# Numerators copied out of PSUM by ScalarE and divided by GpSimd, in an attention, mixture and FFN kernel on one core

## The reference

```
def phi(x):                                  # x: [4 batches, 8 heads, 576 tokens, 64]
    proj = einsum('bhsd,df->bhsf', x, w_phi) # 128 features
    proj = proj - max(abs(proj), -1)
    return concatenate([exp(proj), exp(-proj)], -1)
q_p, k_p = phi(q), phi(k)
kv, z = einsum('bhsf,bhsd->bhfd', k_p, v), sum(k_p, 2)
num = einsum('bhsf,bhfd->bhsd', q_p, kv)
den = einsum('bhsf,bhf->bhs', q_p, z) + 1e-6
x = num / den                                # 2304 tokens x 512
e = argmax(x @ w_gate)                       # one of 8 experts for each token
x = softmax weight * sigmoid(x @ w_output_gate)[e] * (relu(x @ w1[e]) @ w2[e])
x = x / rms(x) * rms_g
out = (silu(x @ w_gate2) * (x @ w_val)) @ w_out
```

## Time and profile before

| | us |
|---|---|
| runs | 900.57, 896.76, 899.69 (median 899.69) |
| the profiled execution | 903.42, span 901.8 |
| TensorE busy, matmuls | 874.1 (97% of the span) |
| VectorE busy | 432.3 (48%) |
| ScalarE busy | 294.0 (33%) |
| GpSimd busy | 123.2 (14%) |

### The profile page before, as it was taken

The page is one execution under the profiler, slowest core; times in us unless marked ns, Lnnn a source line. Parts: engine busy times, 40 slices in busy tenths (PEclk is TensorE's granted clock), DMA queues, the critical chain, the costliest instruction groups (busy, mean ns, idle before and its releaser), DMA issues.

```text
span 901.8 us, 16710 instructions
## 1 busy us (share of the span) xinstructions
PE 874.1 (97%) x6432; PEld 792.1 (88%) x6433; DVE 432.3 (48%) x875; ACT 294.0 (33%) x479; POOL 123.2 (14%) x145
## 2 busy tenths in 40 slices
PE   8999999998999999999999999999999999999996
PEld 6776858678999999999989999999999999999996
DVE  5687787988586444433457422222222222222222
ACT  4555444662255433223354221121121112112111
POOL 1010202023244211224300010010001001001001
PEclk9999999999999999999999999999999999999999
DMA  8614614012637443237633520030020002000000
GB/s 285 194 54 183 216 52 156 3 54 55 250 129 155 80 64 73 57 42 182 146 121 137 160 104 1 1 105 1 1 70 35 0 14 91 0 0 36 1 1 36
DMA packets 37185, 75.37 MB, mean 84 GB/s; under 512 B 8176, under 2 KB 24688, under 8 KB 35472
## 3 DMA queue, kind: packets, MB, share of 16 engines
q1 hardware_dynamic: 32832, 56.07, 23.0%
q0 software_dynamic: 3488, 17.85, 5.3%
q10 hardware_dynamic: 816, 0.79, 0.3%
HBM read 51.06 MB, written 23.64 MB: 83 GB/s over the span
## 4 chain that ended last, share of the span: by engine, by line
PE 83%; DVE 7%; DMA 4%; issue 3%; ACT 2%; POOL 0%; POOLq 0%; SPq 0%; DVEq 0%; ACTq 0%
PE ps L1026 10%; PE ps L1028 10%; PE ps L1027 10%; PE ps L1041 5%; PE ps L1042 5%; PE ps L1040 5%; PE ps L928 3%; PE ps L941 3%; PE ps L929 3%; PE ps L930 3%; PE ps L943 3%; PE ps L942 3%; PE ps L769 3%; PE ps L824 3%; PE ps L729 2%
## 5 line engine op out<-in xcount | busy, mean ns | idle before, releaser
L1026 PE MATMUL ps<-xnH,blkH 128*128 128x384 f32 x576 | 193.7, 336 | 3.0 <-DVE blkL L1693 1.9
L1028 PE MATMUL ps<-xnH,blkL 128*128 128x384 f32 x576 | 193.4, 336 | 0.0
L1027 PE MATMUL ps<-xnL,blkH 128*128 128x384 f32 x576 | 193.2, 335 | 0.0
L1700 DVE TENSOR_TENSOR sg<-sg,ps 128x384 f32<-128x384 f32 x72 | 39.8, 553 | 245.1 <-ACT sg L1259 245.1
L1259 ACT ACTIVATE sg<-ps 128x384 f32<-128x384 f32 x72 | 35.4, 491 | 251.8 <-PE ps L1028 251.8
L1026 PEld LDWEIGHTS ps<-xnH,blkH 128*128 128x128 f32 x576 | 108.2, 188 | 7.1 <-issue 4.4
L1027 PEld LDWEIGHTS ps<-xnL,blkH 128*128 128x128 f32 x576 | 108.2, 188 | 2.7
L1028 PEld LDWEIGHTS ps<-xnH,blkL 128*128 128x128 f32 x576 | 108.1, 188 | 0.0
L1041 PE MATMUL ps<-blkL,hH 128*128 128x512 f32 x216 | 84.8, 393 | 0.0
L1042 PE MATMUL ps<-blkH,hL 128*128 128x512 f32 x216 | 84.8, 392 | 0.0
L1040 PE MATMUL ps<-blkH,hH 128*128 128x512 f32 x216 | 84.5, 391 | 0.0
(11 more groups left out here) (219 smaller groups left out, 1553.8 us busy)
## 6 DMA issues: line engine op xcount, KB each, us to landing
stage<-in_ffn_w SPq DMA_DIRECT2D x12, 768.0 KB, 4.3
xin<-xs_dram SPq DMA_DIRECT2D x9, 578.2 KB, 9.5
xs_dram<-zrow SPq DMA_DIRECT2D x8, 578.2 KB, 8.6
qT<-in_q SPq DMA_DIRECT2D x4, 1152.0 KB, 5.8
xnH_dram<-xoH SPq DMA_DIRECT2D x8, 576.0 KB, 3.5
xnL_dram<-xoL SPq DMA_DIRECT2D x8, 576.0 KB, 5.4
xnH<-xnH_dram SPq DMA_DIRECT2D x6, 768.0 KB, 4.9
xnL<-xnL_dram SPq DMA_DIRECT2D x6, 768.0 KB, 6.3
```

Source lines behind the costliest of these rows:

```text
L1026: e.matmul(o, hi, xnH[par][:, c, :], start=(c == 0), stop=False)
L1027: e.matmul(o, hi, xnL[par][:, c, :], start=False, stop=False)
L1028: last = e.matmul(o, lo, xnH[par][:, c, :], start=False, stop=(c == KC - 1))
```

## The change

`x5` goes; `x5n` holds the 81 values of each head for two tiles, in SBUF, and `rd` becomes double, too. The four full tiles of a batch are copied out of PSUM by ScalarE; the packed tile by VectorE. GpSimd multiplies by the reciprocal where it copied before. Each tile waits until the tile two before it has been divided. The early step's flag comes one slot earlier, its rows are loaded once the last batch's key projections (not its query projections) are through, and GpSimd gates them between Q0 and Q1 of the last batch.

```diff
+            def copy_numerators(at):                      # ScalarE
+                j = at[1] % NJ
+                e.wait_ge(s["pe_N"], nkq(at))
+                if not (isinstance(at[0], int) and at[0] == 0 and j < 2):
+                    e.wait_ge(s["pool_x"], aside_of(two_before(at)))
+                    e.wait_ge(s["dve_lp"], nkq(two_before(at)))
+                e.activation(x5n[:, j % 2, :, :].rearrange("p (b h) e -> p b (h e)", b=2),
+                             num_of(at).rearrange("p b h e -> p b (h e)"), ACT.Copy)\
+                    .then_inc(s["act_N"], 1)
...
             def slot(b, sl):                              # ScalarE
...
+                g2 = before_slot(b, sl, 2)
+                full = is_q(g2) and not packed(g2)
+                if full and is_q(g1):
+                    copy_numerators(g2)
                 if is_k(g1):
...
                 if is_q(g1):
...
                     e.wait_ge(s["pe_pT"], nkq(g1))
                     e.activation(ex[:, g1[1] % 2, 0, heads, :], PMT[:, heads, :], ACT.Exp)
                     e.activation(ex[:, g1[1] % 2, 1, heads, :], PMT[:, heads, :], ACT.Exp, scale=-1.0)\
                         .then_inc(s["act_Q"], 1)
+                if full and not is_q(g1):
+                    copy_numerators(g2)
...
             def normalise(at):                            # VectorE
+                if not (isinstance(at[0], int) and at[0] == 0 and j < 2):
+                    e.wait_ge(s["pool_x"], aside_of(two_before(at)))
+                if packed(at):
+                    e.wait_ge(s["pe_N"], nkq(at))
+                    e.wait_ge(s["dve_lp"], nkq(two_before(at)))
+                    e.tensor_copy(x5n[:, j % 2, 0:HALF, :], num_of(at)[:, 0, :, :]).then_inc(s["dve_N"], 1)
+                    e.wait_ge(s["dve_N"], at[0] + 1)
+                else:
+                    e.wait_ge(s["act_N"], nfull(at))
...
-                e.tensor_tensor(x5[:, j, 0:heads * D].rearrange("p (b h d) -> p b h d", b=banks, d=D),
-                                num[:, :, :, 0:D], r4.unsqueeze(3).to_broadcast([P, banks, 4, D]), ALU.mult)\
-                    .then_inc(s["dve_N"], 1)
...
             def set_aside(b, j):                          # GpSimd
-                e.wait_ge(s["dve_N"], b * NJ + (j + 1))
+                e.wait_ge(s["dve_rd"], nkq(at) * 2)
-                    e.tensor_copy(x5s[0:n, j, 0:DM], x5[0:n, j, :]).then_inc(s["pool_x"], 1)
+                    e.tensor_tensor(x5s[:, j, 0:DM].rearrange("p (h d) -> p h d", d=D), x5n[:, j % 2, :, 0:D],
+                                    rd[:, j % 2, :].unsqueeze(2).to_broadcast([P, H, D]), ALU.mult)\
+                        .then_inc(s["pool_x"], 1)
...
-            for j in range(2):
-                set_aside(B - 1, j)
+            set_aside(B - 1, 0)
             e.wait_ge(s["r_early"], 1)
             with e.If(early > 0):
                 gate_rows(0)
-            for j in range(2, NJ):
+            for j in range(1, NJ):
                 set_aside(B - 1, j)
...
-                e.wait_ge(s["pe_P"], B * 2 * NS)          # SyncE, ahead of the early rows
+                e.wait_ge(s["pe_P"], (B - 1) * (2 * NS) + 2 * NJ)
...
-                    e.wait_ge(s["dve_N"], at[0] * NJ - 1) # TensorE, ahead of a batch's first key sums
+                    e.wait_ge(s["act_N"], at[0] * (NJ - 1))
-                        e.wait_ge(s["dve_N"], nkq((at[0], at[1] - 2)))  # and of numerators
+                        e.wait_ge(s["act_N"], nfull((at[0], at[1] - 2)))
...
-                if isinstance(b, int) and (b, sl) == (B - 1, 8):        # VectorE
+                if isinstance(b, int) and (b, sl) == (B - 1, 7):
                     route_early()
```

More of the change, by code:

```diff
@@ L96, in build_program @@
         kvs = att("kvs", [P, KC, 4, VA])
-        x5 = att("x5", [P, NJ, DM])
+        x5n = att("x5n", [P, 2, H, VA])
         x5s = att("x5s", [P, NJ, ROW])
@@ L171, in build_program @@
         mx = sb("mx", [P, 2, H])
-        rd = sb("rd", [P, H])
+        rd = sb("rd", [P, 2, H])
         lg = sb("lg", [P, NJ, 2 * E])
@@ L231, in build_program @@
                 "act_kv dve_kv pe_C act_cv dve_cv",
-            "queries: transposed, features, numerators, 1 / denominators, rows; logits by head, logits":
-                "pe_pT act_Q pe_N dve_rd dve_N dve_lp dve_g dve_L",
+            "queries: transposed, features, numerators, on chip, 1 / denominators; logits by head, logits":
+                "pe_pT act_Q pe_N act_N dve_N dve_rd dve_lp dve_g dve_L",
             "routing: steps, experts, exponentials, ranks, ranks read, places": "r_chain r_hot r_exp pe_R r_evac r_pos",
-            "rows set aside, scattered, their buffers free": "pool_x scat c_vec",
+            "rows normalised, scattered, their buffers free": "pool_x scat c_vec",
             "the early step's flag, its steps; the table": "r_early e_chain tab_set",
@@ L309, in nkq, with nfull @@
             return at[0] * NJ + (at[1] % NJ + 1)
+        def nfull(at):
+            return at[0] * (NJ - 1) + (at[1] % NJ + 1)
         def num_of(at):
@@ L314, in num_of, with two_before, aside_of @@
             return ps[:, first:first + 2, 0:4 * VA].rearrange("p b (h e) -> p b h e", e=VA)
+        def two_before(at):
+            j = at[1] % NJ
+            return (at[0], at[1] - 2) if j > 1 else (at[0] - 1, NS - 1 - j)
+        def aside_of(at):
+            return at[0] * (NJ + 1) + (NJ + 1 + at[1] % NJ + 1 + packed(at))
         def settle(eng, name):
@@ L591, in set_aside @@
             def set_aside(b, j):
-                n = rows_of(j)
-                e.wait_ge(s["dve_N"], b * NJ + (j + 1))
+                at = (b, NJ + j)
+                e.wait_ge(s["dve_rd"], nkq(at) * 2)
                 settle(e, "carry_pool")
-                if j < NJ - 1:
-                    e.tensor_copy(x5s[0:n, j, 0:DM], x5[0:n, j, :]).then_inc(s["pool_x"], 1)
-                else:
-                    e.wait_ge(s["pool_x"], b * (NJ + 1) + (NJ + 1 + j))
-                    settle(e, "carry_pool")
[L600 to L604, removed]
+                if not packed(at):
+                    e.tensor_tensor(x5s[:, j, 0:DM].rearrange("p (h d) -> p h d", d=D), x5n[:, j % 2, :, 0:D],
+                                    rd[:, j % 2, :].unsqueeze(2).to_broadcast([P, H, D]), ALU.mult)\
+                        .then_inc(s["pool_x"], 1)
+                    return
+                e.wait_ge(s["pool_x"], b * (NJ + 1) + (NJ + 1 + j))
+                settle(e, "carry_pool")
+                for g in range(2):
+                    rows = rows_half(g)
+                    e.tensor_tensor(x5s[0:REM, j, g * HALF * D:(g + 1) * HALF * D].rearrange("p (h d) -> p h d", d=D),
+                                    x5n[rows, j % 2, 0:HALF, 0:D], rd[rows, j % 2, 0:HALF].unsqueeze(2)
+                                    .to_broadcast([REM, HALF, D]), ALU.mult).then_inc(s["pool_x"], 1)
+                    e.wait_ge(s["pool_x"], b * (NJ + 1) + (NJ + 1 + j + 1 + g))
+                    settle(e, "carry_pool")
             def scatter(b):
@@ L772, in key_sums @@
                 if j == 0 and not first:
-                    e.wait_ge(s["dve_N"], at[0] * NJ)
+                    e.wait_ge(s["dve_N"], at[0])
                     settle(e, "carry_pe")
@@ L980, in _ @@
                 hidden(0, 0, 1)
-                e.wait_ge(s["dve_N"], B * NJ)
+                e.wait_ge(s["dve_N"], B)
                 hidden(0, 0, 2)
@@ L1095, in tile_high @@
                 e.activation(tH[sl % 2][:, :, 0:rows_of(sl % NJ)], tile_of(at), ACT.Copy).then_inc(s["act_x"], 1)
+            def copy_numerators(at):
+                j = at[1] % NJ
+                e.wait_ge(s["pe_N"], nkq(at))
[5 more added lines that the diff above has]
+                    .then_inc(s["act_N"], 1)
             def turned_evac(b, i):
@@ L1347, in normalise @@
             def normalise(at):
[L1348 to L1351, removed]
+                j, heads = at[1] % NJ, HALF if packed(at) else H
+                num, r = x5n[:, j % 2, 0:heads, :], rd[:, j % 2, 0:heads]
+                if not (isinstance(at[0], int) and at[0] == 0 and j < 2):
+                    e.wait_ge(s["pool_x"], aside_of(two_before(at)))
@@ L1352, in normalise @@
+                if packed(at):
[5 more added lines that the diff above has]
+                    e.wait_ge(s["act_N"], nfull(at))
                 if j > 0:
-                    e.wait_ge(s["dve_N"], nkq(at) - 1)
                     e.wait_ge(s["dve_L"], nkq(at) - 1)
@@ L1355, in normalise @@
                 links = (nkq(at) - 1) * 2
-                r4 = rd[:, 0:heads].rearrange("p (b h) -> p b h", b=banks)
-                e.tensor_scalar(r4, num[:, :, :, VW], 1e-6, None, ALU.add).then_inc(s["dve_rd"], 1)
+                e.tensor_scalar(r, num[:, :, VW], 1e-6, None, ALU.add).then_inc(s["dve_rd"], 1)
                 e.wait_ge(s["dve_rd"], links + 1)
-                e.reciprocal(rd[:, 0:heads], rd[:, 0:heads]).then_inc(s["dve_rd"], 1)
```

(6 more changed lines are left out.)

## The result

The changed kernel takes 932.66 us (median of 4 runs, 930.42 to 935.62), the kernel before 898.95: ratio 1.0378, 95% interval 1.0354 to 1.0402, slower by 33.7 us. The forecast was 923.8, in a range from 916 to 932: the sign was right, the loss over a quarter too small.

A forecast was written before the change was run, and what follows sets the result against it. TensorE was taken to bound the query part, VectorE some microseconds at the turns. 18.0 us for three turns plus 6.1 in the last batch gave 24.1: 927.5 profiled, 923.8 us unprofiled, range 916 to 932.

The forecast's parts named there:

- The ring: Query slots: numerators, ScalarE copy, exponentials and transposes await each other; 18.0 us over three turns, 6.1 in the last batch.
- E + 2.73: Next transposes start 2.73 us after E, the end of a tile's numerators: signals, copy and two exponentials lie between.
- Stalls of 1.98, 1.93, 1.98: Lateness in us of the transposes of Q2, Q3 and Q4 in each batch; together 5.9 a batch.
- 3.5 for Q4's numerators: TensorE waits about 1 us for Q4's exponentials before its numerators; mostly covered by VectorE's lag at the turn.
- The clock: TensorE's granted clock stays at 1.00, its upper level, through the new idle gaps; nothing added to the sum.
- rival 4: Repeated idle gaps in query slots drop TensorE's clock to 1.2 GHz: at most +54 us, half of it +27, 951; 6%.
- the clock shows below 1.00 there: Sign that the forecast is wrong: TensorE's granted clock under its full level at the query transposes' idle gaps.
- Rival 1: Query slots: numerators are finished when ScalarE reaches the copy, so no wait is added; −6.1 us, 893.6; 6%.
- Rival 2: Q4's 1.98 us stall vanishes in VectorE's lag at three query-to-key turns: 18.2 instead of 24.1, 917.9; 15%.
- Rival 3: GpSimd's multiplies slow VectorE at the turns from queries to keys: +3.3 us, 927.1; 13%.
- VectorE's relief: VectorE loses a 0.60 us multiply on each of sixteen full tiles, packed tile even; buys nothing beyond the turns' sum.
- The early rows: Last batch: rows gated earlier, so TensorE's 2.47 us wait for them goes, but waits for exponentials fill it.

The follow-up runs named there:

- the second chip: Changed kernel run again against the kernel before, both on another chip than the first measurement: ratio 1.0358.
- the added wait alone: Kernel before plus one wait: ScalarE's query exponentials wait for the previous tile's numerators, nothing copied; ratio 1.0164 to the kernel before.
- the rows and sums moved: Kernel before with the early-rows change, and VectorE's numerator multiply and logit sum moved behind the first maxima and next low part; ratio 1.0077.

## Why the prediction was wrong

- *The ring* was right in kind and size. Forecast: transposes at E + 2.73; measured 163.37 − 160.60 = 2.77. Stalls of 1.98, 1.93, 1.98: measured 1.87, 1.92, 1.97 in the third batch. 2.80 in the last: 2.73. The copy 0.71 long: 0.711 on the mean. As a net sum the forecast was 24.1. On the second chip the waits for exponentials are 27.8, the wait for early rows is 2.4 less and the other waits at the turns are 1.8 less: 23.6. (Of the 3.5 for Q4's numerators, which the turns were to cover, those 1.8 came back.)
- *The clock* is the step that failed. The sum put the lower clock at nothing: it held TensorE at its upper level, on the reading of one gap, and gave rival 4 6%; "the clock shows below 1.00 there" was among its own signs of being wrong. The spells add 8.5 us on the second chip (seven instead of two). With them the forecast 24.1 becomes 32.6, against 33.3 measured there; without them the loss would be 24.8, inside the range. Rival 4 named the mechanism but mis-sized it as well: 27 to 54 us, as if whole query parts ran at half speed; it is spells of some 3.4 us, 1.7 us each, at a third to a half of the gaps. The reading of the earlier trace rows is the error that can be named: the gap of 2.5 us showed 1.00, and in that trace the clock stayed there; in the second trace of the same kernel the same gap showed 1.00 and a spell began 1 us behind it. So neither the clock read inside a gap nor one trace of it shows what follows. In the changed kernel the first gap and what follows it read so:
```profile
45.50:47.20 1.70, 0.00 (x0) 0.00 (x1) 1.49 (x6) 1.65 (x2) 1.05 (x1) 1.00 0.00 0
47.20:48.20 1.00, 1.00 (x8) 0.86 (x8) 0.68 (x1) 0.00 (x0) 0.00 (x0) 1.00 0.00 0
48.20:51.70 3.50, 3.50 (x39) 3.16 (x38) 0.00 (x0) 0.00 (x0) 0.00 (x0) 0.57 0.00 0
```
  The Trainium skill, "TensorE: Matmul & The Clock Gate", section "HAM oscillation — how this bites in real kernels", describes a kernel in which each of many idle gaps lets the clock drop again. The trace agrees in kind, with gaps of 1.7 to 2.0 us; but the gaps of the page's kernel are longer, and here not each of them was followed by a drop. The prediction had cited the page and set it aside on the reading of one gap.
- *Rival 1* (hidden) is out: the added wait alone costs 14.9 us. *Rival 2* (the turn absorbs the third stall) is out: the 1.97 are there, and the turn behind them is not shorter: 30.0 us where it has no spell (from 121.18 to 151.19), against 29.4 before (from 106.30 to 135.70). *Rival 3*: GpSimd's multiply took 1.05 us, between the bounds of 0.94 and 2.11; whether it slows VectorE at the turns was not tested by itself.
- *VectorE's relief* was counted as 0.6 a tile and the packed tile as even; it is 0.44, less a later start, and −0.39 for the packed one: a loss of 0.6 a turn. It is small beside the rest. The estimate that the two small reads get 0.06 us shorter out of SBUF is not borne out: the one of the denominators takes 0.179 us on the mean out of SBUF, 0.159 out of PSUM.
- *The early rows* were right: in time, and without effect behind the ring. By themselves they give 3.4 us, where the wait that they remove is 2.5.

## What to carry to other kernels

Ahead of putting work on an engine with slack, ask what that engine waits for at that place, and whether its next output is awaited by the engine that it would wait for: a short copy ahead of an awaited operation turns two overlapped streams into one ring. When such a ring leaves TensorE idle a few times in a row, price the clock as well, from stretches behind gaps, not inside them, and from more than one trace of the same kernel. And a relief of the bounding engine is read between its neighbours in the list, not from the length of the instruction that goes.

## What the runs showed of the hardware that was not expected

- Gaps of 1.7 to 2.0 us (2.7 for the last), three in 15 to 17 us, were followed by the clock at 1.2 GHz in four to six places of twelve, and in none when matmuls filled them; in the one trace with gaps of 1.1 to 1.2 us in the same places, no spell began behind one of these. With the rows and sums moved, TensorE's single gaps of 2.1 us ahead of the key sums were not followed by one either; the one of 3.8 us was, by one of double length. Which of the gaps is followed by one changes from run to run: in the first four runs of the changed kernel the mean clock goes from 0.988 to 0.983 and the time from 930.4 to 935.6 us. The clock falls late: in the busy stretch up to some 1.5 us behind the gap, or at the gap's very end.
- From the second batch on, TensorE stands idle inside Q0's numerators while the profile shows nothing that it waits for ("issue"): 3.7 us in 9 brackets in the first trace of the kernel before, 5.2 in the second, none in the first trace of the changed kernel, 3.7 and 5.1 in its others. In nine of the thirteen traces that have it, at least one of these places is followed by a spell. It costs more than its brackets: in the first trace of the kernel before it takes 4.9 us from Q1's transposes to Q2's in the first batch and 6.9 to 7.2 in the others. That the first trace of the changed kernel lacks it is one reason why the two profiled executions lie closer together than the medians. Why it comes, and why not in that one, stays open; no run tested it. Busy DMA engines alone are not the reason: their share is 0.95 where it comes (the changed kernel on the second chip, 100 to 102 us) and 0.96 where it does not (its first trace, at the same time).
